# mLSTM and two MLPs on one core: tile addresses, three multiplications on GpSimd, factors at a step's end, chunks 5 to 11 one step earlier

## The reference

```python
for t in range(S):                              # S = 768, for every batch and head
    m_new = maximum(f[t] + m, i[t])
    f_stab, i_stab = exp(f[t] + m - m_new), exp(i[t] - m_new)
    m = m_new
    C = f_stab * C + i_stab * outer(v[t], k[t])
    n = f_stab * n + i_stab * k[t]
    y[t] = sigmoid(o[t]) * (C @ q[t]) / maximum(abs(n @ q[t]), 1)
x = y as (1536, 320)
h = x @ w_in                                    # 2048 wide
x = (h - tanh(h)) @ w_out
out = sum over e of p[:, e:e+1] * (maximum(x @ w1[e], 0) @ w2[e])   # 4 experts, 1024 wide
```

## Time and profile before

| | |
|---|---|
| median of 3 runs | 598.75 us (597.57 to 599.56) |
| profiled execution | 597.8 us |
| its span, first to last instruction | 596.1 us |
| mean granted TensorE clock | 0.997 |
| TensorE busy | 586.9 us (98%) |
| VectorE busy | 237.2 us (40%) |
| ScalarE busy | 201.0 us (34%) |
| GpSimd busy | 104.1 us (17%) |

### The profile page before, as it was taken

How to read it: one execution, slowest core, us unless ns; L and a number is a source line. 1 busy time by engine, 2 the same in 40 slices (tenths; PEclk the granted TensorE clock), 3 DMA queues, 4 the chain that set the end, 5 groups by cost and what they waited for, 6 DMA issues and landing times.

```text
span 596.1 us, 8943 instructions
## 1 busy us (share of the span) xinstructions
PE 586.9 (98%) x3660; PEld 531.9 (89%) x3660; DVE 237.2 (40%) x474; ACT 201.0 (34%) x396; POOL 104.1 (17%) x75
## 2 busy tenths in 40 slices
PE   8999999999999999999999999999999999999998
PEld 7899999989988888899999999999999999999997
DVE  6566757676655333413132313131323131323222
ACT  5675645555534444611113311113311111111111
POOL 3868201111000244420003400004400000000000
PEclk9999999999999999999999999999999999999999
DMA  6978544554220133210001210001000000001011
GB/s 252 347 241 279 221 111 134 169 158 112 58 50 27 38 98 104 93 58 0 1 1 48 98 49 1 1 1 48 1 0 1 2 0 1 1 0 45 1 44 46
DMA packets 35343, 43.84 MB, mean 74 GB/s; under 512 B 18670, under 2 KB 27878, under 8 KB 35302
## 3 DMA queue, kind: packets, MB, share of 16 engines
q1 hardware_dynamic: 35302, 43.26, 22.6%
HBM read 38.85 MB, written 4.40 MB: 73 GB/s over the span
## 4 chain that ended last, share of the span: by engine, by line
PE 90%; DVE 5%; issue 1%; DMA 1%; SPq 1%; ACT 1%; DVEq 0%
PE bank L1125 10%; PE bank L1126 10%; PE bank L1124 10%; PE bank L1175 9%; PE bank L1176 9%; PE bank L1174 9%; PE bank L1128 5%; PE bank L1127 5%; PE bank L1145 4%; PE bank L1147 3%; PE bank L1146 3%; PE bank L1153 1%; PE bank L1154 1%; PE bank L963 1%; PE bank L974 1%
## 5 line engine op out<-in xcount | busy, mean ns | idle before, releaser
L940 DVE SCALAR_TENSOR_TENSOR g_lo<-bank,g_hi 128x512 fp32r<-128x512 f32 x96 | 66.3, 691 | 254.2 <-ACT g_hi L659 254.2
L659 ACT ACTIVATE g_hi<-bank 128x512 fp32r<-128x512 f32 x96 | 57.5, 599 | 270.5 <-PE bank L1128 270.4
L1175 PE MATMUL bank<-w_all,g_hi 128*128 128x320 f32 x384 | 118.8, 309 | 0.0
L1176 PE MATMUL bank<-w_all,g_lo 128*128 128x320 f32 x384 | 118.6, 309 | 0.0
L1124 PE MATMUL bank<-x_hi,w_all 128*128 128x512 f32 (+2 forms) x318 | 117.2, 369 | 1.3 <-DVE x_hi L841 1.3
L1174 PE MATMUL bank<-w_all,g_hi 128*128 128x320 f32 x384 | 118.5, 309 | 0.0
L1126 PE MATMUL bank<-x_hi,w_all 128*128 128x512 f32 (+2 forms) x318 | 118.4, 372 | 0.0
L1125 PE MATMUL bank<-x_lo,w_all 128*128 128x512 f32 (+2 forms) x318 | 118.3, 372 | 0.0
L480 POOL TENSOR_TENSOR w_all<-w_raw,w_all 128x1408 fp32r<-128x1408 f32 x16 | 51.6, 3227 | 232.6 <-ACT w_all L542 232.6
L1175 PEld LDWEIGHTS bank<-w_all,g_hi 128*128 128x128 f32 x384 | 72.2, 188 | 3.8
L1174 PEld LDWEIGHTS bank<-w_all,g_hi 128*128 128x128 f32 x384 | 72.2, 188 | 3.7
(11 more groups left out here) (134 smaller groups left out, 644.0 us busy)
## 6 DMA issues: line engine op xcount, KB each, us to landing
w_raw<-in_w SPq DMA_DIRECT2D x24, 704.0 KB, 4.1
feat<-in_feat SPq DMA_DIRECT2D x12, 512.0 KB, 4.7
tok<-in_tok SPq DMA_DIRECT2D x12, 484.0 KB, 5.6
zb<-z SPq DMA_DIRECT2D x10, 512.0 KB, 4.5
out<-arena SPq DMA_DIRECT2D x12, 160.0 KB, 1.9
spare<-xg SPq DMA_DIRECT2D x7, 256.0 KB, 2.6
fb<-f SPq DMA_DIRECT2D x14, 80.0 KB
xg<-feat SPq DMA_DIRECT2D x14, 80.0 KB
```

The costliest lines, as they stand in the source:

```text
L659: A(g_hi[:, b, 0:N], h_ps[b][:, 0:N], ACT.Relu).then_inc(ghi_ready, 1)
L940: V.scalar_tensor_tensor(g_lo[:, b, 0:N], h_ps[b][:, 0:N], 0.0, g_hi[:, b, 0:N].bitcast(F32), ALU.max, ALU.subtract).then_inc(g_ready, 1)
L1175: mm(out, g_hi[:, b, t], low_w, start=False, stop=False)
L1176: last = mm(out, g_lo[:, b, t], high_w, start=False, stop=stop)
```

## The change

- The `sb(...)` calls are reordered: `tok` comes last, and `g_tmp`, `g_hi`, `g_lo`, `tails` directly behind `x_lo`. Sizes are the same. All tiles then begin at a multiple of 64 bytes; `w_all`, `w_raw`, `x_hi` and `x_lo` keep their place.
- Chunks 5 to 11 begin one step earlier.
- `scale_q`, `decay_state` (of chunks 5 to 11) and `gate_x` run on GpSimd, which also does `cut_z` and `weigh_v` one chunk further ahead in its order.
- `factors` stands behind the step's `g_lo`. `finish_state` waits for a new semaphore `state_less`, which GpSimd's decay raises.

```diff
-START = {2: 3, 3: 7, 4: 10, 5: 15, 6: 19, 7: 23, 8: 27, 9: 31, 10: 35, 11: 39}
+START = {2: 3, 3: 7, 4: 10, 5: 14, 6: 18, 7: 22, 8: 26, 9: 30, 10: 34, 11: 38}
...
+            def scale_q(n):
+
+                q = feat[0:KP, n % RING, 0:PAIRS * CH].rearrange("p (j t) -> p j t", t=CH)
+                pool.wait_ge(fb_in, 32 * (n - FEAT + 1))
+                pool.wait_ge(s_ready, n + 1)
+                G.tensor_tensor(q, q, fb[0:KP, :, :], ALU.mult).then_inc(q_scaled, 1)
+
+            def decay_state(n):
+                own, r0 = state[0:KP, n % 2, :, :, 0:HDE], row0(n)
+                pool.wait_ge(inter_ready, n - 1)
+                pool.wait_ge(beta_ready, 1)
+                pool.wait_ge(state_ready, n)
+                G.tensor_tensor(own, own, two(spread(beta[0:KP, r0:r0 + HEADS], HDE)), ALU.mult).then_inc(state_less, 1)
+
+            def gate_x(n):
+                pool.wait_ge(xg_in, 48 * (n - FEAT + 1))
+                G.tensor_tensor(xg[:, :, 0, :], xg[:, :, 0, :], xg[:, :, 1, :], ALU.mult).then_inc(x_gated, 1)
...
-            for n in range(5, STEPS):
+            weigh_v(FEAT)
+            cut_z(FEAT + 1)
+            for n in range(FEAT, STEPS):
+                scale_q(n)
+                decay_state(n)
+                if n > FEAT:
+                    gate_x(n - 1)
+                if n + 2 < STEPS:
+                    cut_z(n + 2)
                 if n + 1 < STEPS:
-                    cut_z(n + 1)
-                weigh_v(n)
+                    weigh_v(n + 1)
+            gate_x(STEPS - 1)
...
                 dve.wait_ge(sums_ready, n + 1)
                 chain.wait()
+                after(dve, state_less, n - FEAT + 1)
...
-                        if k == FACTORS and n >= FEAT:
-                            factors(n)
                     dve.wait_ge(ghi_ready, m + 1)
                     V.tensor_tensor(g_lo[:, b, 0:N], h_ps[b][:, 0:N], g_hi[:, b, 0:N].bitcast(F32),
                                     ALU.subtract).then_inc(g_ready, 1)
                     for n, k in phase(m):
                         if k == 1:
                             scores(n, 1, b_ps)
-                            if n >= FEAT:
-                                scale_q(n)
-                        if k == SUMS:
-                            finish_sums(n) if n < FEAT else decay_state(n)
-                        if k == GATED and n >= FEAT:
-                            gate_x(n)
+                        if k == SUMS and n < FEAT:
+                            finish_sums(n)
+                        if k == FACTORS and n >= FEAT:
+                            factors(n)
                         if k == SUMS + 1:
```

More of the change, by code:

```diff
@@ L53 @@
 L1_STEPS = len(L1_SIZES) * L1_TILES
-START = {2: 3, 3: 7, 4: 10, 5: 15, 6: 19, 7: 23, 8: 27, 9: 31, 10: 35, 11: 39}
+START = {2: 3, 3: 7, 4: 10, 5: 14, 6: 18, 7: 22, 8: 26, 9: 30, 10: 34, 11: 38}
 FEAT = 5
 SUMS, TURN = 2, 4
-FACTORS, GATED, FEAT_TURN = 4, 7, 8
+FACTORS, FEAT_TURN = 4, 8
 GRP = 4 * CH
@@ L119, in mlstm_mlp_experts @@
         x_lo = sb("x_lo", [P, 2, TOK], F32R)
-        spare = sb("spare", [P, 6 * P])
-        yt = spare[:, 0:2 * D].rearrange("p (r d) -> p r d", d=D)
-        xg = spare[:, :].rearrange("p (k g t) -> p k g t", k=3, g=2)
-        ident = sb("ident", [P, P])
-        probs = sb("probs", [P, STEPS, EXPERTS])
-        tok = sb("tok", [P, RING, 3 * D + HEADS])
-        feat = sb("feat", [P, RING, 2 * PAIRS * CH])
-        zb = sb("zb", [P, 2, HEADS, CH])
-        wa = sb("wa", [P, 3, ROWS])
-        fb = sb("fb", [P, PAIRS, CH])
-        state = sb("state", [P, BATCH, PAIRS, 2, 64])
-        dn = state[:, 0, 0, 1, 64 - HEADS:64]
+        g_tmp = sb("g_tmp", [P, 2, GRP])
+        g_hi = sb("g_hi", [P, 2, GRP], F32R)
+        g_lo = sb("g_lo", [P, 2, GRP], F32R)
+        tails = sb("tails", [P, 2, GRP])
+        tail = tails[0:TAIL, :, :]
         arena = sb("arena", [P, STEPS * D])
@@ L145, in mlstm_mlp_experts @@
         out_acc = arena[:, 0:STEPS * D].rearrange("p (n d) -> p n d", d=D)
-        g_tmp = sb("g_tmp", [P, 2, GRP])
-        g_hi = sb("g_hi", [P, 2, GRP], F32R)
-        g_lo = sb("g_lo", [P, 2, GRP], F32R)
-        tails = sb("tails", [P, 2, GRP])
-        tail = tails[0:TAIL, :, :]
+        zb = sb("zb", [P, 2, HEADS, CH])
+        feat = sb("feat", [P, RING, 2 * PAIRS * CH])
+        fb = sb("fb", [P, PAIRS, CH])
+        state = sb("state", [P, BATCH, PAIRS, 2, 64])
+        dn = state[:, 0, 0, 1, 64 - HEADS:64]
+        spare = sb("spare", [P, 6 * P])
+        yt = spare[:, 0:2 * D].rearrange("p (r d) -> p r d", d=D)
+        xg = spare[:, :].rearrange("p (k g t) -> p k g t", k=3, g=2)
+        ident = sb("ident", [P, P])
+        probs = sb("probs", [P, STEPS, EXPERTS])
+        wa = sb("wa", [P, 3, ROWS])
+        tok = sb("tok", [P, RING, 3 * D + HEADS])
         early = g_tmp[0:ROWS, :, :].rearrange("p b c -> p (b c)")
@@ L188, in mlstm_mlp_experts @@
         q_scaled = sem("q_scaled")
+        state_less = sem("state_less")
         sums_out = sem("sums_out")
@@ L785, in finish_sums @@
                 rows_out(n, c_ps)
-                decay_state(n)
-            def decay_state(n):
-                own, r0 = state[0:KP, n % 2, :, :, 0:HDE], row0(n)
-                dve.wait_ge(inter_ready, n - 1)
+                own = state[0:KP, n % 2, :, :, 0:HDE]
                 dve.wait_ge(beta_ready, 1)
@@ L802, in finish_state @@
                 last.then_inc(state_ready, 1)
-            def scale_q(n):
-                q = feat[0:KP, n % RING, 0:PAIRS * CH].rearrange("p (j t) -> p j t", t=CH)
-                dve.wait_ge(fb_in, 32 * (n - FEAT + 1))
-                dve.wait_ge(s_ready, n + 1)
-                V.tensor_tensor(q, q, fb[0:KP, :, :], ALU.mult).then_inc(q_scaled, 1)
             def factors(n):
@@ L827, in factors @@
                 V.transpose(tok[:, r, 0:D], o).then_inc(factors_turned, 1)
-            def gate_x(n):
-                dve.wait_ge(xg_in, 48 * (n - FEAT + 1))
-                V.tensor_tensor(xg[:, :, 0, :], xg[:, :, 0, :], xg[:, :, 1, :], ALU.mult).then_inc(x_gated, 1)
             def by_row(t_ps):
```

## The result

The changed kernel takes **593.25 us** (median of 5 runs, 592.2 to 597.5), the kernel before took 598.34 beside it (5 runs, 597.6 to 599.6). The ratio is 0.9919, 95% interval 0.9897 to 0.9942: 0.8% faster, 3.5 to 6.2 us. The forecast was 594.0, a gain of 4.7 us.

The account below looks back on a forecast made before the run. Bound: TensorE's stream, decided by its waits for VectorE in the first MLP layer up to step 48. 5.3 us gone, 0.6, 0.1 and 0.2 come, 0.3 from addresses: 4.7 us gained, 594.0 us; range 591 to 597.

Parts of the forecast that it names:

- what goes: First MLP layer up to step 48: TensorE's waits for `g_lo` and `x_hi`, restarts and one scaled-q wait vanish, 5.3 us.
- The new wait behind chunk 11: No scores follow there, so `factors` at step 42's end delays `down(43)`: 0.5 us, 0.6 with its restart.
- GpSimd's operations: Moved multiplications stay hidden from TensorE: `scale_q` 1.3 us, `decay_state` 0.8 to 1.0, `gate_x` 0.9 to 1.1.
- The clash: Late divisors make VectorE's `factors` meet GpSimd's `scale_q` in chunks 7 to 9; 0.2 us put in the sum.
- rival 1: That clash exceeds its cover in two or three chunks, 1.2 to 1.8 us: 595.2 to 595.8, up to 597; chance 0.18.
- I take 0.4: Cost of one VectorE and GpSimd meeting, from `gate_x` at 0.94 against 0.55 us; at most `scale_q`'s whole 1.3.
- the loop of 14.9 us: The divisors' way through `factors` and DMAs takes 14.9 us a chunk, against 15.0 for four TensorE steps.
- a wait of TensorE lengthens the period and heals it: Argument against lateness persisting in the divisors' loop: TensorE's own waiting lets it catch up; no size given.
- The addresses: `g_hi` and `g_lo` move to multiples of 64 bytes: 0.3 us gain taken, bounds 2.6 gained to 0.6 lost.
- rival 2: Expert down matmuls slow down from the new `g_hi`, `g_lo` place: 9.2 us at 8 ns each, about 603.5; chance 0.06.
- if the spacing of the experts' matmuls moves: Sign that the prediction is wrong: it expected the expert stage to stay as long as it is.
- rival 3: Chunks 7 and 11: `x_low` waits for GpSimd's `gate_x`, so 1.6 us of group-start waits stay: 595.7; chance 0.04.

Follow-up runs that it names:

- e12: The changed kernel with chunks 5 to 11 beginning at their old steps (15, 19, ... 39): 593.43 us, ratio 0.993.
- e9: The changed kernel with only the f load moved behind the divisors on SyncE's queue, z staying first: 589.71 us, ratio 0.9859.
- e2: The changed kernel with the old tile order, so without the address change: 597.3 us, ratio 0.998.
- e10: The changed kernel with `g_tmp`, `g_hi`, `g_lo`, `tails` at multiples of 64 bytes and all tiles behind them 32 bytes off: 594.5 us, ratio 0.994.
- e11: The changed kernel with only `g_tmp`, `g_hi`, `g_lo` and `tails` 32 bytes off a multiple of 64: 594.7 us, ratio 0.994.
- e1: The kernel before with only the new tile order: 595.83 us against 598.65, ratio 0.9944.
- e3: The changed kernel run once more, unaltered: 593.9 us, ratio 0.9909 to the kernel before.
- e8: The changed kernel with the old tile order, the same program as e2, run once more: 596.74 us, ratio 0.997.

## Why the prediction was right, and where it was not

The time was right (594.0 against 593.25) by luck: two misses, of 4.2 and 2.8 us, cancel in large part, and the clocks at the start gave the medians about another microsecond. Point by point:

- **What bounds the kernel, and what goes (5.3 us): right.** The six waits for `g_lo` and the two at group starts are absent from both profiles of the changed kernel, and e12 brings back the two that belong to the begin of the chunks, at 2.2 us with what comes with them where 1.6 was in the sum. e9, where nothing else waits, measures the term: its stage in chunks is 6.1 us shorter than before's. Of that 1.1 is the spacing (e2's 119.03, less 1.3 for its one wait, against e9's 116.65), so 5.0 us are waits, where 5.3 less the new wait of 0.4 makes 4.9.
- **The new wait behind chunk 11 (0.6): right.** In the changed kernel `down(43)` starts 0.46 us after the last matmul of its up sweep where 0.17 is the spacing, and takes 0.44 instead of 0.33: 0.4 us.
- **GpSimd's operations: right.** `scale_q` took 1.28 us (1.3 in the working), `decay_state` 0.74 (0.8 to 1.0, so a little less), `gate_x` 1.01 (0.9 to 1.1).
- **The clash (0.2 in the sum, 1.2 to 1.8 as rival 1 at a chance of 0.18): mis-sized, 4.4 us.** Three steps of the working failed. The first is "I take 0.4" for a meeting, from `gate_x` at 0.94 against 0.55. There 0.53 us of GpSimd's cut were left when `gate_x` began; here `scale_q` begins just before VectorE's second operation, which is held to its end, 0.97 us on one of 0.17. The Trainium skill ("SBUF — State Buffer", Who interferes with whom) says that who issues first has the shared pair of SBUF ports for the whole instruction; these rows agree, and the 1.3 us end of the prediction was the right one to take. The second is the loop of 14.9 us, read from one round. The round before it in the same trace took 13.9 us from the end of `factors` at 97.50 to the landing at 111.42, which with 1.7 makes 15.6, and the changed kernel had 13.9 again: longer than the old period and 0.8 more than the new one, before any meeting. The third is "a wait of TensorE lengthens the period and heals it". With a `factors` of 2.7 the loop is 16.6 against 14.8, so three chunks pay 1.2 to 1.5 us each, where rival 1 had 0.6 in two or three. Late z adds to it: the cut and the weighing meet `x_low` as well, which the prediction did not have. Against e9 the stage in chunks is 4.4 us longer (121.03 less 116.65). I had written "up to 597 if it also feeds the loop" and left it out of the price. Four steps of 15.0 against a loop of 14.9 should have been read as a second bound: whoever takes TensorE's waits away makes SyncE's queue the next limit.
- **The addresses (0.3 in the sum, 2.6 at most): mis-sized, 3.1 us.** Group 4 gave 1.4 (63.08 in e2 against 61.66; a further 0.1 of before's 63.20 is the restart after its wait), the steps of 384 columns 1.1, the rest 0.6. The bound was too low because it let only the sweeps over `g` gain, from 1.88 to the 1.84 of x. The sweep over x was taken as undisturbed and wasn't: both went to 1.81. What is read from the same disturbed execution is no floor. "Half, since nothing shows yet that the address is its cause" was caution in the wrong place; the edit says that it moves just these tiles, and the row was there. The Trainium skill's rule of 16-byte lines, cited in the prediction ("SBUF — State Buffer", DMA port swizzle), gives zero, and e10 against e11 contradicts that for this kernel.
- **Experts (rival 2): did not happen.** The load of `g` as weights has the same 188 ns, the stage is 0.6 us shorter, not longer. The prediction called itself wrong "if the spacing of the experts' matmuls moves", and it moved: 3.593 us a step instead of 3.600. That was the address term again (e1, which changes addresses alone, has 3.593 too, e11 3.600), in a stage to which the prediction gave nothing.
- **x late at group starts (rival 3): did not happen.** No wait for `x_hi` in either profile.

The sum made again: 5.0 of waits gone (the new one taken off), 3.1 of addresses, 0.1 of the restart in group 4, 4.4 of meetings and late divisors come: 3.8 us less. The two profiles have 3.6 and 3.8 us from the first sweep on, the runs at an equal clock about 4, the medians 4.8 to 5.1. The about 1 us between them fits the clock at the start: two of e3's six runs have a mean clock of 1.0, none of the 17 of before beside it.

## What to carry to other kernels

When the waits of the bounding engine are taken away, look for the loop that has next to no slack: add up one round of a DMA queue and the work that closes it, and compare it with the shorter period, not with the old one; take the longest round in the trace, not one of them. A store whose result comes back from memory goes ahead of loads that have a step to spare, but behind the one that another engine's queue waits for: one load, ahead of the divisors or behind them, is about 4 us of 593 here (e9 against the changed kernel: 588.9 to 589.0 against 592.9 to 593.5 us, all at a mean clock of 0.997). And where two tiles are the same kind of operand and read at a different spacing, try the address first; it is a line to change, and here its gain counted in every step of 384 and 512 columns. Where runs differ in the clock they were granted at the start, compare runs of one clock, or stages of the traces.

## What the runs showed of the hardware

- Eight matmuls of 512 columns over `g` take 1.87 to 1.88 us with the `g` tiles and `tails` 32 bytes off a multiple of 64 and 1.81 to 1.82 at a multiple; eight over x, whose own place is the same, 1.84 to 1.85 and 1.81 to 1.82. The cause within the chip isn't shown.
- A VectorE operation of 8 elements a partition took 1.14 us instead of 0.17 when a GpSimd multiplication of 1.28 us had begun 0.18 us before it. GpSimd's weighing took 0.90 us beside VectorE's `x_low` (changed) and 0.74 alone (e9).
- The same program had one such meeting that TensorE waited for in one execution (593.5 us, e2) and four in another (598.8 us, e8).
- The first sweep of one and the same program began at 17.52 us with a granted clock of 1.00 in the first 20 us and at 22.32 with 0.79. Of the 50 runs of before that stand beside e1 to e12, those with mean clocks of 0.997, 0.994 and 0.991 (45 in all) took 597.4, 598.8 and 600.4 us on average.
